# The order of the first four chunks of a fused attention and MLP kernel, written out by hand

## The reference

```python
# 1. attention: q, k, v of (4, 8, 576, 64), a causal window of 64 keys
scores = q @ k.T / sqrt(64); scores = where(0 <= i - j < 64, scores, -1e9)
attn = exp(scores - max); attn = attn / (sum + 1e-9); x = attn @ v      # x: 2304 x 512
# 2. first MLP, 512 -> 1536 -> 512
xn = x / sqrt(mean(x*x) + 1e-6) * rms_g
g = xn @ w_gate; x2 = (g * sigmoid(g) * (xn @ w_val)) @ w_out
# 3. second MLP, 512 -> 2048 -> 512
h = x2 @ w_in; out = (h * sigmoid(1.702 * h)) @ w_out2
```

## Time and profile before

| | before |
|---|---|
| median of three runs | 902.53 us |
| profiled execution, its own time | 902.16 us |
| its span, first to last instruction | 900.4 us |
| TensorE busy | 887.5 us (99%) |
| VectorE, ScalarE (ACT), GpSimd (POOL) busy | 540.4, 400.6, 82.2 us |
| TensorE clock granted | 1.000 |

### The profile page before, as it was taken

The page is one execution under the profiler, slowest core; times in us unless marked ns, Lnnn a source line. Parts: engine busy times, 40 slices in busy tenths (PEclk is TensorE's granted clock), DMA queues, the critical chain, the costliest instruction groups (busy, mean ns, idle before and its releaser), DMA issues.

```text
span 900.4 us, 14698 instructions
## 1 busy us (share of the span) xinstructions
PE 887.5 (99%) x5368; PEld 769.3 (85%) x5368; DVE 540.4 (60%) x1256; ACT 400.6 (44%) x944; POOL 82.2 (9%) x111
## 2 busy tenths in 40 slices
PE   8899999999999999999999999999999999999998
PEld 7799888888888888888888899999999999999997
DVE  6997533334343344333346578887788788877663
ACT  6766333342333433334123354545464554545442
POOL 5144001030011300112000000000000000000000
PEclk9999999999999999999999999999999999999999
DMA  7672111102111021100400221121432121241201
GB/s 243 214 227 89 51 51 51 50 24 74 51 50 55 20 74 50 51 25 8 179 1 24 94 99 66 68 73 47 164 118 94 48 79 63 70 142 48 70 24 71
DMA packets 41079, 69.77 MB, mean 77 GB/s; under 512 B 3632, under 2 KB 13872, under 8 KB 41008
## 3 DMA queue, kind: packets, MB, share of 16 engines
q1 hardware_dynamic: 39600, 67.12, 23.0%
q10 hardware_dynamic: 1408, 1.70, 0.6%
HBM read 59.38 MB, written 9.44 MB: 76 GB/s over the span
## 4 chain that ended last, share of the span: by engine, by line
PE 95%; ACT 2%; DVE 1%; issue 1%; DMA 0%; POOL 0%; SPq 0%; POOLq 0%; DVEq 0%; ACTq 0%
PE ps L647 16%; PE ps L649 16%; PE ps L648 16%; PE ps L839 7%; PE ps L840 7%; PE ps L838 7%; PE ps L781 7%; PE ps L777 7%; PE ps L779 6%; PE ps L628 2%; PE ps L600 2%; PE ps L614 2%; ACT prob L881 1%; DMA wstage<-in_w_a 0%; ACT xT L881 0%
## 5 line engine op out<-in xcount | busy, mean ns | idle before, releaser
L647 PE MATMUL ps<-x_hi,w_all 128*128 128x512 f32 (+1 forms) x480 | 179.4, 374 | 0.6 <-issue 0.5
L649 PE MATMUL ps<-x_lo,w_all 128*128 128x512 f32 (+1 forms) x480 | 176.7, 368 | 0.0
L648 PE MATMUL ps<-x_hi,w_all 128*128 128x512 f32 (+1 forms) x480 | 176.7, 368 | 0.0
L840 PE MATMUL ps<-w2out,hB 128*128 128x512 f32 x288 | 113.0, 392 | 0.0
L839 PE MATMUL ps<-w2out,hB 128*128 128x512 f32 x288 | 112.9, 392 | 0.0
L838 PE MATMUL ps<-w2out,hB 128*128 128x512 f32 x288 | 112.0, 389 | 0.0
L647 PEld LDWEIGHTS ps<-x_hi,w_all 128*128 128x128 f32 x480 | 90.4, 188 | 19.0 <-issue 3.9
L649 PEld LDWEIGHTS ps<-x_lo,w_all 128*128 128x128 f32 x480 | 90.4, 188 | 15.2
L648 PEld LDWEIGHTS ps<-x_hi,w_all 128*128 128x128 f32 x480 | 90.5, 188 | 14.5
L1254 DVE SCALAR_TENSOR_TENSOR sig<-sig,ps 128x512 f32<-128x512 f32 x48 | 32.9, 686 | 107.1 <-ACT sig L996 107.1
L647 PE MATMUL ps<-h_hi,w_all 128*128 128x512 f32 (+1 forms) x240 | 89.8, 374 | 1.9 <-DVE hid L1263 1.6
(11 more groups left out here) (148 smaller groups left out, 1555.6 us busy)
## 6 DMA issues: line engine op xcount, KB each, us to landing
wstage<-in_w_b SPq DMA_DIRECT2D x48, 512.0 KB, 3.7
wstage<-in_w_a SPq DMA_DIRECT2D x36, 256.0 KB, 3.5
vwin<-in_v_win SPq DMA_DIRECT2D x32, 256.0 KB, 3.7
kwin<-in_k_t SPq DMA_DIRECT2D x32, 160.0 KB, 3.5
x2raw<-x_scratch SPq DMA_DIRECT2D x3, 1536.0 KB, 6.6
out_dram<-yB SPq DMA_DIRECT2D x18, 256.0 KB, 4.3
qtok<-in_q_t SPq DMA_DIRECT2D x34, 128.0 KB, 2.6
x_scratch<-wstage SPq DMA_DIRECT2D x3, 1024.0 KB, 4.2
```

What stands on the lines that cost most here:

```text
L647: pe.matmul(out_, w[:, 0, cols], xh, start=first, stop=False, **flags)
L648: pe.matmul(out_, w[:, 1, cols], xh, start=False, stop=False, **flags)
L649: return pe.matmul(out_, w[:, 0, cols], xl, start=False, stop=last, **flags)
L840: ins = pe.matmul(y, hB_of(g, chunk, 1)[:, rows], w[:, 0, chunk, :], start=False, stop=last)
```

## The change

Four streams get another order in the first four chunks of tile 0; no instruction is added or dropped, and the arithmetic is the same.

- **VectorE:** the loop over chunks 0 to 3 is replaced by a list. `silu_A` and `hidden_A` of chunk 1 move ahead of `weights_lo_A(1, 2)`, (2, 2), (3, 0) and (3, 1); `row_max(4)`, the splits of (3, 0) and (3, 1), and `row_max(5)` follow, then reciprocal and normalisation of step 4, and only then the split of (1, 2). The splits of (2, 2), (4, 0), (4, 1) come next, (3, 2) after `hid_lo_A(0, 2)`, (4, 2) and (5, 2) last.
- **ACT:** the exponentials of steps 4 and 5 stand together, ahead of the casts of (4, 0) and (4, 1); then the copies of transposed probabilities, tanh of chunk 2, the casts of (5, 0) and (5, 1), the cast of hidden chunk 2, tanh and cast of chunk 3, and the casts of (6, 0), (6, 1).
- **TensorE:** `project_A(0, 1)` stands between the transposes of steps 4 and 5, no longer behind both.
- **SP:** behind (3, 0), (3, 1), (3, 2) come (4, 0), (4, 1), q and k of steps 6 and 7, then (5, 0), (5, 1), (4, 2), (5, 2), then chunk 6 as before.

```diff
-        FIRST_SPLITS = ((0, 0), (0, 1), (1, 0), (1, 1), (2, 0), (0, 2), (2, 1), (1, 2), (2, 2))
+        FIRST_SPLITS = ((0, 0), (0, 1), (1, 0), (1, 1), (2, 0), (0, 2), (2, 1), (3, 0), (3, 1), (1, 2),
+                        (2, 2), (4, 0), (4, 1), (3, 2), (5, 0), (5, 1), (4, 2), (5, 2))
...
-            return FIRST_SPLITS.index((c, m)) + 1 if c < 3 else 3 * c + m + 1
+            return FIRST_SPLITS.index((c, m)) + 1 if c < 6 else 3 * c + m + 1
... SP
-                    if t == 0 and c + 3 < CA:
+                    if (t, c) == (0, 1):
+                        load_wA(4, 0)
+                        load_wA(4, 1)
+                        load_step_qk(EARLY + 2)
+                        load_step_qk(EARLY + 3)
+                    elif (t, c) == (0, 2):
+                        load_wA(5, 0)
+                        load_wA(5, 1)
+                        load_wA(4, 2)
+                        load_wA(5, 2)
+                    elif t == 0 and c + 3 < CA:
                         for m in range(3):
                             load_wA(c + 3, m)
... TensorE
                         transpose_probs(transposed)
+                    if (t, c) == (0, 3):
+                        project_A(t, c - LAG)
+                    if transposed is not None:
                         transpose_probs(transposed + 1)
-                    if c >= LAG:
+                    if c >= LAG and (t, c) != (0, 3):
                         project_A(t, c - LAG)
... ACT
+            tanh_A(0, 0)
+            tanh_A(0, 1)
+            hid_hi_A(0, 0)
+            weights_hi_by_act(3, 0)
+            weights_hi_by_act(3, 1)
+            hid_hi_A(0, 1)
+            exponentials(EARLY)
+            exponentials(EARLY + 1)
+            weights_hi_by_act(4, 0)
+            weights_hi_by_act(4, 1)
+            copy_probT(EARLY)
+            copy_probT(EARLY + 1)
+            tanh_A(0, 2)
+            weights_hi_by_act(5, 0)
+            weights_hi_by_act(5, 1)
+            hid_hi_A(0, 2)
+            tanh_A(0, 3)
+            hid_hi_A(0, 3)
+            weights_hi_by_act(6, 0)
+            weights_hi_by_act(6, 1)
... VectorE
+            scale_gate(0)
+            scale_gate(1)
+            weights_lo_A(2, 1)
+            silu_A(0, 0)
+            hidden_A(0, 0)
+            silu_A(0, 1)
+            hid_lo_A(0, 0)
+            hidden_A(0, 1)
+            row_max(EARLY)
+            weights_lo_A(3, 0)
+            weights_lo_A(3, 1)
+            row_max(EARLY + 1)
+            reciprocal_of_sum(EARLY)
+            normalise(EARLY)
+            weights_lo_A(1, 2)
+            hid_lo_A(0, 1)
+            reciprocal_of_sum(EARLY + 1)
+            normalise(EARLY + 1)
+            scale_gate(2)
+            weights_lo_A(2, 2)
+            weights_lo_A(4, 0)
+            silu_A(0, 2)
+            hidden_A(0, 2)
+            weights_lo_A(4, 1)
+            hid_lo_A(0, 2)
+            weights_lo_A(3, 2)
+            scale_gate(3)
+            weights_lo_A(5, 0)
+            silu_A(0, 3)
+            hidden_A(0, 3)
+            weights_lo_A(5, 1)
+            hid_lo_A(0, 3)
+            weights_lo_A(4, 2)
+            weights_lo_A(5, 2)
+
             for t in range(NA):
-                for c in range(CA):
+                for c in range(4 if t == 0 else 0, CA):
```

More of the change, by code:

```diff
@@ L450, in _ @@
                 for c in range(CA):
-                    if t == 0 and c + 3 < CA:
+                    scored = pair_with_scores_at(t, c - 1)
+                    multiplied = pair_with_scores_at(t, c - 3)
+                    if (t, c) == (0, 1):
[9 more added lines that the diff above has]
+                    elif t == 0 and c + 3 < CA:
                         for m in range(3):
                             load_wA(c + 3, m)
-                    scored = pair_with_scores_at(t, c - 1)
-                    multiplied = pair_with_scores_at(t, c - 3)
-                    if scored is not None and scored + 2 < STEPS:
+                    if scored is not None and scored + 2 < STEPS and (t, c) != (0, 2):
                         load_step_qk(scored + 2)
@@ L1027, in _ @@
                         copy_probT(transposed + 1)
[L1028 to L1031, removed]
+                    tanh_A(t, c)
                     if c == SUMSQ_AT and t + 1 < NA:
@@ L1293, in _ @@
                     split = c + 2 if t == 0 and c + 2 < CA else None
-                    if t == 0 and c != 1:
+                    if t == 0:
                         scale_gate(c)
-                    if t == 0 and c == 0:
-                        scale_gate(1)
-                        weights_lo_A(2, 1)
                     if scored is not None:
@@ L1301, in _ @@
                         normalise(scored)
-                    if split is not None and c > 0 and c != 2:
+                    if split is not None:
                         weights_lo_A(split, 0)
@@ L1315, in _ @@
                         normalise(scored + 1)
-                    if split is not None and c == 2:
-                        weights_lo_A(split, 0)
-                    if split is not None and c > 0:
+                    if split is not None:
                         weights_lo_A(split, 1)
-                    if t == 0 and c == 0:
-                        weights_lo_A(1, 2)
                     hid_lo_A(t, c)
```

## The result

The changed kernel takes 908.36 us (median of six runs, 907.84 to 908.96), the kernel before 902.93 us in the same comparison: 5.4 us slower, ratio 1.0064, 95% interval 1.0053 to 1.0074. The forecast was +4.4 us. One execution each of three kernels further down took 2.28 to 2.48 ms, for which nothing measured here gives a reason; the ratios leave them out, and the medians move by less than 0.1 us without them.

What follows compares the result with a forecast made beforehand. TensorE, busy at full clock, bounds the kernel, with the loop split, load, cast nearly as late between 20 and 60 us. The legs less what is given back made +4.7, taken as +4.4 on 902.53: 906.9 us, range 904 to 910.5.

Steps and rivals of the forecast that it cites:

- The waits removed: TensorE, chunks 1 to 3: waits of 1.64, 0.99 and 1.56 us go, putting it 4.5 us ahead.
- First leg: Late split of (1, 2) delays the load of (4, 1) and `probs_by_v(4)`: lead of 4.5 us becomes lag of 0.9.
- Second leg: Late split of (3, 2) delays chunk 6's loads and ACT's output copy: `val(0, 4)` at 47.8, shift +5.2 us.
- The sum: Whole kernel: +4.7 us with both loads at 4.04, taken as +4.4, giving 906.9 us.
- rival (c): TensorE's clock falls in two idle stretches of 5.5 and 4.6 us: 2.9 us more, 909.8 us; chance 0.20.
- the prediction's own sign: TensorE's granted clock under 1.00 in the slices of 35 to 60 us was to mean rival (c).
- the forecast with the full clock: Whole kernel slower by 4.4 us with TensorE's clock at 1.00: 906.9 us; chance 0.52.
- What is given back: Behind `val(0, 4)`, at `val(0, 6)` with 0.46 us idle before it: TensorE's lag drops to ACT's, +4.75 us.
- (a): Rival, faster: loads in chunks 0 to 3 aren't late enough to matter, stalls go; -2, 900.5 us; chance 0.15.
- (b): Rival, no change: short landings in both legs, VectorE's stream 1 to 1.5 us shorter; 902.5 to 903; chance 0.07.
- (d): Rival: only the first leg counts, TensorE lags by 0.9 us behind `probs_by_v`; 903.4 us; chance 0.06.

Runs made afterwards that it cites:

- parts alone: Kernel before, with only silu_A and hidden_A of chunk 1 moved up and project_A(0, 1) between the transposes: 902.59 us against 902.97.
- other buffers: Changed kernel with pieces (3, 2), (4, 0), (4, 1) loaded into free memory (rinv, part of xT), orders kept: 903.06 us against 902.73.
- second profile: The changed kernel run and profiled again with nothing changed, used as a check; its span is 905.3 us.
- slowest try: Normalisation of steps 4 to 11 on POOL, added to other buffers with ACT and VectorE reordered: 911.79 us against 902.99.

## Why the prediction was right, and which terms were off

**The waits removed.** Right: all three are gone, `project_A(0, 0)` without a wait. One sentence on it was wrong: that a shift of TensorE in this stretch goes to the end one for one. A lead does not. The kernel with these parts alone ends where the kernel before does (902.59 against 902.97), and of the 4.0 us of lead with other buffers 0.3 us is left at `val(0, 4)`. Of a lag, most goes on (below).

**First leg.** Right. The split of (1, 2) ended at 32.7, less 0.83 is 31.9 (said: 31.65). The load of (4, 1) took 3.57 us, not 4.04, and `probs_by_v(4)` began at 39.2 (said: 39.6), behind `hidden_A(0, 2)`.

**Second leg.** Right in its path: `val(0, 4)` at 47.9 (said: 47.8), so TensorE's shift is +5.3 there (said: +5.2), and the copy out by ACT released it. That the number fits to 0.1 us is luck: in the second profile `val(0, 4)` starts at 47.1, a shift of +4.5. And one of the signs did not come: the second wait was to be 4 to 6 us long, and was 2.8 us (3.15 in the second profile), because TensorE came to it later, at the low clock.

**The sum.** The shift by rows was +4.7 behind the exponentials, and I took +4.4, for a shorter load in the first leg. That load was 0.5 us shorter; but the cast of hidden chunk 2, behind ACT's casts of chunk 5, ended at 41.4 without the offset and not at 40.45, and the last load took 3.1 and not 4.04. The terms of the legs were off by up to 0.9 us with both signs and cancelled; to take off 0.3 was a choice without ground. The estimate of 2.6 us for a load is below all of these: the Trainium skill, "DMA: Bandwidth & Descriptors", has it in the section "Anatomy of one DMA — SWDGE (gpsimd) path", so for DMAs issued from GpSimd, and here SP issues them.

**The clock, rival (c).** It did fall, twice, and I had given that 0.20. By the prediction's own sign what happened is (c), and not the forecast with the full clock; the measured 908.36 us lies between the 906.9 of the one and the 909.8 of the other. (c)'s mechanism was right; its price was not. I said 2.9 us more. In the profile the 12 matmuls of `val(0, 4)` took 2.7 us (48.76 to 51.46), before 1.5 (42.62 to 44.13): 1.2 us more, and behind them the clock was back; what was slow ahead of that was covered, as said. In the second profile the low stretch came later, from 48.5 to 51.9, in `project_A(0, 2)` and `gate(0, 5)`, and cost 1.5 us. So the term is 1.2 to 1.5 us, and the medians with idle matmuls could not tell it. The Trainium skill, page "TensorE: Matmul & The Clock Gate", section "What's actually happening", says that the half rate is the default and activity releases it; this trace agrees (0.53 in the stretch behind the wait of 4.75 us).

**What is given back.** TensorE's shift, profile against profile, is 7.4 us at the transposes of steps 6 and 7 (55.82 against 48.45) and 6.5 at those of 8 and 9 (67.62 against 61.15): 0.9 back, where I said 0.46 at `val(0, 6)`, and 0.2 more until the end. So 0.83 + 5.3 + 1.2 - 1.1 = 6.2 us, and the spans differ by 6.3; without the chance 0.83 that is 5.5, and the runs say 5.4. The second profile adds up in the same way from other terms: 4.5 + 1.5 - 1.1 = 4.9 us, and its span is 4.9 us longer than before (905.3 against 900.4). By the first profile the measured excess over the forecast is thus the low clock less what was given back beyond the forecast, and the 0.3 us taken off.

**The rivals.** (a) failed as argued against it: the loads weren't there. Its price of -2 us is not borne out either: with other buffers they are there, and the time is 903.06 against 902.73. (b) and (d) failed with the second leg: ACT's copy ends 0.1 us ahead of `val(0, 4)`, and with the copy moved ahead of the casts that wait is gone.

## What to carry to other kernels

Where a load goes into a buffer that another engine must free, and several loads share one queue, an instruction that frees a buffer has a due time of its own: that of everything queued behind the load, not that of its own result. "By need" of the result, (1, 2) was not due before `project_A(0, 1)`; by need of SP's queue it was due before `row_max(4)`: moved there, it gave back 4.2 us. Before reordering a stream, write down for each wait what is queued behind it on that engine, and follow that once round the loop; and read 4.9 of 5 us busy on the helper engine as a sign that a lead of the main engine may not last.

## What the runs showed of the hardware that was not expected

- Behind a wait of 2.18 us TensorE ran at the lower clock in the kernel with the parts alone (0.70 granted from 35 to 40 us; its four transposes at 34.61 took 1.11 us, and 0.66 in the earlier trace rows), while behind waits of 1.91 and 2.02 us in the kernel with other buffers the clock was 1.00.
- In the same changed kernel the low clock met other matmuls from profile to profile: behind the wait of 2.82 us all of `val(0, 4)` was slow, behind that of 3.15 us `val(0, 4)` ran at 0.12 us a matmul and what follows was slow.
- With idle matmuls in both waits the clock stayed full through 2.3 and 2.4 us of idle time left over.
- At the lower clock matmuls of 256 columns started every 0.21 us, at the full clock every 0.12: less than twice as far apart.
- The same load of 256 KB, third of three, took from 3.1 to 4.7 us in kernels that differ only in idle matmuls; that is more than most of the effects here.
- A normalisation of 128 x 512 took 1.04 us on POOL in three of four cases ahead of tile 0, and 1.16 to 1.40 beside VectorE's full stream. In the slowest try, with VectorE busy for 0.05 of 5 us, two took 2.04 us together.
